# Attention scores from queries and keys split on VectorE, three single-pass products per pair of heads, keys in a ring

## The reference

```python
scores = q @ k.T / sqrt(64)                     # batch 2, 8 heads, 768 positions, head_dim 64
keep = (key < 4) | ((query - key >= 0) & (query - key < 128))
a = softmax(where(keep, scores, -1e9)); x = a @ v     # -> 1536 tokens x 512
x = moe_top2(x)     # 8 experts, 512 -> 1024 -> 512, noisy top-2 routing
x = moe_top1(x)     # 8 experts, 512 -> 1024 -> 512, top-1 routing
```

## Time and profile before

| what | value |
|---|---|
| median of 3 runs | 675.39 us |
| the profiled execution | 674.08 us, its span 672.0 us |
| TensorE busy | 639.0 us, 95% |
| VectorE busy | 329.8 us, 49% |
| ScalarE busy | 275.7 us, 41% |
| granted clock of TensorE over the span | 0.99 |
| attention stage | about the first 132 us |

### The profile page before, as it was taken

The page is one execution under the profiler, slowest core; times in us unless marked ns, Lnnn a source line. Parts: engine busy times, 40 slices in busy tenths (PEclk is TensorE's granted clock), DMA queues, the critical chain, the costliest instruction groups (busy, mean ns, idle before and its releaser), DMA issues.

```text
span 672.0 us, 11238 instructions
## 1 busy us (share of the span) xinstructions
PE 639.0 (95%) x3866; PEld 580.1 (86%) x3867; DVE 329.8 (49%) x681; ACT 275.7 (41%) x529; POOL 184.7 (27%) x199
## 2 busy tenths in 40 slices
PE   7989999899999999999999999999988999999981
PEld 6989999898999999999999999988767888788871
DVE  4466645588365526254361634467876222542220
ACT  5667866442344335252443523144516123522110
POOL 2500100117362533516144251201652121121010
PEclk9999999999999999999999999999998999999996
DMA  7867822263684646646355520724649211001000
GB/s 209 281 235 240 291 74 80 66 249 74 237 214 138 132 148 157 190 142 156 111 122 177 148 28 3 171 63 159 171 138 387 102 48 47 20 32 48 16 32 11
DMA packets 51089, 89.84 MB, mean 134 GB/s; under 512 B 7919, under 2 KB 14063, under 8 KB 51040
## 3 DMA queue, kind: packets, MB, share of 16 engines
q1 hardware_dynamic: 41872, 69.21, 31.0%
q0 software_dynamic: 9168, 19.97, 13.3%
HBM read 73.13 MB, written 17.02 MB: 134 GB/s over the span
## 4 chain that ended last, share of the span: by engine, by line
PE 82%; DVE 6%; DMA 3%; ACT 3%; issue 2%; SPq 1%; ACTq 0%; POOL 0%; DVEq 0%; POOLq 0%
PE banks L1060 6%; PE banks L1059 6%; PE banks L999 6%; PE banks L1078 6%; PE banks L1001 6%; PE banks L998 6%; PE banks L803 5%; PE banks L831 4%; PE banks L1377 3%; PE banks L1342 3%; PE banks L1347 3%; PE banks L1343 3%; PE banks L1373 3%; PE banks L1374 3%; PE banks L815 2%
## 5 line engine op out<-in xcount | busy, mean ns | idle before, releaser
L1833 DVE TENSOR_TENSOR split<-stage,split 128x2048 fp32r<-128x2048 f32 x32 | 73.3, 2290 | 41.9 <-ACT split L1463 41.8
L998 PE MATMUL banks<-xTs,split 128*128 128x416 f32 (+1 forms) x256 | 88.6, 350 | 0.0
L999 PE MATMUL banks<-xTs,split 128*128 128x416 f32 (+1 forms) x256 | 86.5, 342 | 0.0
L650 POOL DMA_INDIRECT x_moe<-rows,dst_idx x25 | 49.3, 1971 | 113.2 <-DVE rows L2285 112.2
L1059 PE MATMUL banks<-hTs,split 128*128 128x416 f32 x224 | 79.9, 357 | 0.0
L1060 PE MATMUL banks<-hTs,split 128*128 128x416 f32 x224 | 78.6, 351 | 0.0
L1598 ACT ACTIVATE hTs<-banks 128x416 fp32r<-128x416 f32 x56 | 29.0, 518 | 81.6 <-PE banks L1001 81.6
L1463 ACT ACTIVATE split<-stage 128x2048 fp32r<-128x2048 f32 x32 | 60.9, 1908 | 1.0 <-DMA stage<-w1a 1.0
L1720 ACT ACTIVATE hTs<-banks 128x512 fp32r<-128x512 f32 x28 | 16.5, 596 | 105.8 <-PE banks L1357 105.8
L1001 PE MATMUL banks<-xTs,split 128*128 128x416 f32 (+1 forms) x256 | 56.2, 340 | 0.0
L803 PE MATMUL banks<-k_sb,q_sb 128*128 128x260 f32 (+2 forms) x192 | 49.6, 384 | 3.5 <-DMA k_sb<-k_w 2.1
(11 more groups left out here) (371 smaller groups left out, 1308.3 us busy)
## 6 DMA issues: line engine op xcount, KB each, us to landing
stage<-w1a SPq DMA_DIRECT2D x16, 1024.0 KB, 7.6
stage<-w2a SPq DMA_DIRECT2D x16, 1024.0 KB, 5.4
k_sb<-k_w SPq DMA_DIRECT2D x12, 520.0 KB, 5.0
raw<-w1b SPq DMA_DIRECT2D x4, 1024.0 KB, 7.9
raw<-w2b SPq DMA_DIRECT2D x4, 1024.0 KB, 9.7
q_sb<-q_t SPq DMA_DIRECT2D x24, 128.0 KB, 3.1
x_attention<-rows SPq DMA_DIRECT2D x12, 256.0 KB, 6.1
split<-x_moe SPq DMA_DIRECT2D x12, 256.0 KB, 3.6
```

Of the source, the lines that this page charges most:

```text
L650: pool.indirect_dma_start(out=x_dram[1], out_offset=rows_at(dst_idx[0], early_dst, e, k), in_=y_lines(e, k), in_offset=None, compute_op=AL ...
L998: pe.matmul(psum, piece(slot, 0, o + c * FH), xTs[:, 0, c, 0:cols], start=(c == 0), stop=False)
L999: pe.matmul(psum, piece(slot, 1, o + c * FH), xTs[:, 0, c, 0:cols], start=False, stop=False)
L1833: dve.tensor_tensor(split_chunk(e % 2, 1, c), staged_chunk(e % 2, c), split_chunk(e % 2, 0, c).bitcast(F32), ALU.subtract).then_inc(low_do ...
```

## The change

Only the attention stage and what is loaded or prepared beside it changes.

- Block 0 keeps its fp32 products, on buffers of its own (`q_first`, `k_first`, 128 keys).
- From block 1 on, the scores of a pair are six products: for each of (queries high, keys high), (queries high, keys low) and (queries low, keys high), one product per head with 64 contraction rows. The one head lies in rows 0 to 63 of the array, the other in rows 64 to 127; no zeros are multiplied. The three products of a head add up in PSUM.
- VectorE makes the parts: a cast to fp32r and a subtraction, over 128x512, for the keys and again for the queries of each unit, one such split per odd step, a block ahead.
- The keys lie in a ring of two places of 132 columns (`ODD`), 128 keys and 4 sinks. Block i overwrites the place of block i-2, so only the new 128 keys of a unit are loaded (256 KB, not 520). There is one more mask, since the order of the two places changes with the block.
- A chunk of the first expert's weights is prepared in each of the blocks 2 to 5, not two in each of 2 and 3. Its low part is made in two halves at the steps 2 and 6; the last chunk's at step 6 of block 5 in one piece.
- The loads go to staging buffers and are issued earlier; the zeros are written in the blocks 4 and 5.

```diff
+ODD = P + SINK
+RING = 2 * ODD
...
+        with ExitStack() as first_block:
+            q_first = first_block.enter_context(nc.sbuf_tensor("q_first", [P, BATCH, PAIRS, 2, P], F32))
+            k_first = first_block.enter_context(nc.sbuf_tensor("k_first", [P, BATCH, PAIRS, P], F32))
...
-            k_sb = sb_early("k_sb", [P, BATCH, PAIRS, WIN])
+            k_ring = sb_early("k_ring", [P, BATCH, PAIRS, RING], F32R)
...
-            masks = sb_early("masks", [P, 3, WIN])
+            masks = sb_early("masks", [P, 4, WIN])
+            k_low_ring = sb_early("k_low_ring", [P, BATCH, PAIRS, RING], F32R)
+            q_high = sb_early("q_high", [P, BATCH, PAIRS, P], F32R)
+            q_low = sb_early("q_low", [P, BATCH, PAIRS, P], F32R)
+            q_raw = sb_early("q_raw", [P, BATCH, PAIRS, P])
+            k_raw = sb_early("k_raw", [P, BATCH, PAIRS, P])
...
+        def slot_of(i):
+            return ODD * (i % 2)
+
+        def keys_split(i, b):
+
+            return b + 1 if i == 0 else 2 * BATCH + 4 * i + 2 * b - 3
+
+        def queries_split(i, b):
+            return keys_split(i, b) + 1
...
             def load_unit(i, b):
-                q_unit = qT[bass.ds(i * BATCH + b, 1)].rearrange("a p j n -> (a p) j n")
-                for h in range(2):
-                    own = slice(h * HD, (h + 1) * HD)
-                    sp.dma_start(q_sb[own, b, :, h, :], q_unit[own]).then_inc(qk_in[b], 16)
-                sp.dma_start(k_sb[:, b], kW[bass.ds(i * BATCH + b, 1)].rearrange("a p j n -> (a p) j n")).then_inc(qk_in[b], 16)
+                q_unit, k_unit = qT[i * BATCH + b], kW[i * BATCH + b]
+                if i == 0:
+                    for h in range(2):
+                        own = slice(h * HD, (h + 1) * HD)
+                        sp.dma_start(q_first[own, b, :, h, :], q_unit[own]).then_inc(qk_in[b], 16)
+                    sp.dma_start(k_first[:, b], k_unit[:, :, 0:P]).then_inc(qk_in[b], 16)
+                    return
+                if i == 1:
+                    sp.wait_ge(scores_ready, 4 * b + 1)
+                else:
+                    sp.wait_ge(parts_split, queries_split(i - 1, b))
+                sp.dma_start(k_raw[:, b], k_unit[:, :, P:2 * P]).then_inc(qk_in[b], 16)
+                sp.dma_start(q_raw[:, b], q_unit).then_inc(qk_in[b], 16)
...
-            for i in (1, 2):
+            sp.wait_ge(setup_ready, 11)
+
+            for i in range(1, BLOCKS):
                 for b in range(BATCH):
+                    if i + 1 < BLOCKS:
+                        load_unit(i + 1, b)
                     store_x(i - 1, b)
-                next_block(i + 1)
+                    if b == 0 and i <= CHUNKS:
+                        load_first(sp, 0, i - 1)
...
+                if i == BLOCKS - 2:
+                    zero_rows(0, 8)
+                if i == BLOCKS - 1:
+                    zero_rows(8, TILES + 1)
...
                 b, pair, g = j // PAIRS, j % PAIRS, i * 8 + j
-                if pair == 0:
-                    pe.wait_ge(qk_in[b], i * 48 + 48)
+                if kind == 0 and pair == 0:
+                    pe.wait_ge(qk_in[b], 48)
+                if kind > 0 and pair == 0:
+                    pe.wait_ge(parts_split, queries_split(i, b))
                 if kind > 0 or j >= 2:
                     pe.wait_ge(masked, g * 2 - 2)
-                n = span(kind)
-                for h in range(2):
-                    mm = pe.matmul(S[:, j % 2, h, 0:n], q_sb[:, b, pair, h, :], k_sb[:, b, pair, 0:n], start=True, stop=True)
+                if kind == 0:
+                    for h in range(2):
+                        mm = pe.matmul(S[:, j % 2, h, 0:P], q_first[:, b, pair, h, :], k_first[:, b, pair, :], start=True, stop=True)
+                else:
+                    for n, (queries, keys) in enumerate(((q_high, k_ring), (q_high, k_low_ring), (q_low, k_ring))):
+                        for h in range(2):
+                            own = slice(h * HD, (h + 1) * HD)
+                            if kind == 1:
+                                window = keys[own, b, pair, :].rearrange("p (a n) -> p a n", a=2)[:, :, 0:P]
+                                psum = S[:, j % 2, h, 0:2 * P].rearrange("p (a n) -> p a n", a=2)
+                            else:
+                                window, psum = keys[own, b, pair, 0:WIN], S[:, j % 2, h, 0:WIN]
+                            mm = pe.matmul(psum, queries[own, b, pair, :], window, start=(n == 0), stop=(n == 2))
                 mm.then_inc(scores_ready, 1)
...
+            block_steps(2, 2, 2, {0: 0})
+            block_steps(3, 2, 2, {0: 1})
+            block_steps(4, 2, 2, {0: 2})
+            block_steps(BLOCKS - 1, 2, None, {4: 3})
...
+            def early_weights_low(c, half):
+
+                dve.wait_ge(high_done[c], 1)
+                columns = slice(c * CHUNK + (half == 1) * (CHUNK // 2), (c + 1) * CHUNK - (half == 0) * (CHUNK // 2))
+                low = dve.tensor_tensor(split[:, 0, 1, columns], stage[0][:, columns], split[:, 0, 0, columns].bitcast(F32), ALU.subtract)
+                if half != 0:
+                    low.then_inc(low_done[c], 1)
...
+            def split_keys(i, b):
+
+                at = slice(slot_of(i), slot_of(i) + P)
+                raw_keys = k_raw[:, b] if i else k_first[:, b]
+                if i > 0:
+                    dve.wait_ge(qk_in[b], 16 + 32 * (i + 1))
+                link(dve.tensor_copy(k_ring[:, b, :, at], raw_keys))
+                dve.tensor_tensor(k_low_ring[:, b, :, at], raw_keys, k_ring[:, b, :, at].bitcast(F32), ALU.subtract).then_inc(parts_split, 1)
+
+            def split_queries(i, b):
+                link(dve.tensor_copy(q_high[:, b], q_raw[:, b]))
+                dve.tensor_tensor(q_low[:, b], q_raw[:, b], q_high[:, b].bitcast(F32), ALU.subtract).then_inc(parts_split, 1)
+
+            def sink_keys():
+
+                dve.wait_ge(parts_split, BATCH)
+                dve.tensor_copy(k_ring[:, :, :, P:ODD], k_ring[:, :, :, 0:SINK]).then_inc(parts_split, 1)
+                dve.tensor_copy(k_low_ring[:, :, :, P:ODD], k_low_ring[:, :, :, 0:SINK]).then_inc(parts_split, 1)
...
-                    if pair == 1 and b < len(chunks):
-                        first_layer_low(0, chunks[b])
+                    if i == 0:
+                        if j in (0, 2):
+                            split_keys(0, j // 2)
+                        elif j == 3:
+                            sink_keys()
+                        elif j > 3:
+                            (split_queries if j % 2 else split_keys)(1, (j - 4) // 2)
+                    elif j % 2 and not last:
+                        (split_queries if j // 2 % 2 else split_keys)(i + 1, b)
+                    if j in chunks:
+                        early_weights_low(*chunks[j])
...
+            block_steps(2, 2, 2, {2: (0, 0), 6: (0, 1)})
+            block_steps(3, 2, 2, {2: (1, 0), 6: (1, 1)})
+            block_steps(4, 2, 2, {2: (2, 0), 6: (2, 1)})
...
+            block_steps(BLOCKS - 1, 2, None, {6: (3, None)})
...
```

More of the change, by code:

```diff
@@ L126, in build @@
         xTs = sb("xTs", [P, 2, DC, SLOTS], F32R)
-        with ExitStack() as early:
-            q_sb = early.enter_context(nc.sbuf_tensor("q_sb", [P, BATCH, PAIRS, 2, P], F32))
         hTs = sb("hTs", [P, 2, FC, SLOTS], F32R)
@@ L539, in iota @@
                           allow_small_or_imprecise_dtypes=True).then_inc(const_done, 1)
[L541 to L554 removed]
+            pool.memset(masks[:], 0.0).then_inc(setup_ready, 1)
+            pool.memset(ident[:], 0.0).then_inc(setup_ready, 1)
+            pool.wait_ge(setup_ready, 1)
+            select(masks[:, 0, SINK:P], -SINK, 1, [[-1, P - SINK]], MASKED, setup_ready)
+            pool.wait_ge(setup_ready, 2)
+            select(ident[:], 0, 1, [[-1, P]], 1.0, setup_ready, ALU.not_equal)
+            select(masks[:, 1, SINK:P], SINK - 1, -1, [[1, P - SINK]], MASKED, setup_ready)
+            select(masks[:, 1, P:2 * P], 0, 1, [[-1, P]], MASKED, setup_ready)
+            for odd in range(2):
+                select(masks[:, 2 + odd, ODD * (1 - odd):ODD * (1 - odd) + P], -1, -1, [[1, P]], MASKED, setup_ready)
+                select(masks[:, 2 + odd, ODD * odd:ODD * odd + P], 0, 1, [[-1, P]], MASKED, setup_ready)
+            pool.memset(rows[:, 5, :], 0.0).then_inc(setup_ready, 1)
             pool.memset(before[:], 1.0).then_inc(const_done, 1)
@@ L1510, in early_high_part, with block_steps @@
                                ACT.Copy).then_inc(x1_high, 1)
-            def block_steps(i, kind, next_kind, chunks=()):
+            def block_steps(i, kind, next_kind, chunks={}):
                 for j in range(8):
@@ L1525, in block_steps @@
                         x_copy(*((i, 0) if b else (i - 1, 1)))
-                    if pair == 0 and b < len(chunks):
-                        first_layer_high(0, chunks[b])
+                    if j in chunks:
+                        first_layer_high(0, chunks[j])
```

54 lines of the change are left out of this document (12 added, 42 removed).

## The result

The changed kernel took 701.5 us (median of 4 runs, 697.45 to 704.28) against 676.48 for the kernel before on the same chip (674.67 to 680.53): a ratio of 1.036, 95% interval 1.028 to 1.043. Forecast were 669.0 us and a range up to 680. The profiled execution took 704.28 us, its span is 702.5 (before: 674.08 and 672.0), and the mean granted clock of the span 0.94 where it was 0.99.

A forecast was written before the change was run, and what follows sets the result against it. TensorE was taken to bound the stage, busy all 10.60 us of a block 3 unit. Terms -9.5 + 2.5 + 1.5 - 0.6 - 0.7 = -6.8 us from 674.08 gave 667.3, median about 668.6, stated as 669.0; range 662 to 680.

The forecast's parts named there:

- the clock has nothing to give: Attention stage, block 3 unit: granted clock is 1.00 of the full 2.4 GHz, so no change in clock was priced.
- the slowest rival: Score sets: halves take turns and each shape change waits for the last product's whole record; T 1.05, 683.5 us, chance 0.09.
- T = 0.56 us: A set of scores on TensorE: 0.36 for pairs side by side plus 0.20 for shape changes, instead of 0.915 us.
- rivals 2 and 3: Score halves take turns: 678.1 or 680.7 us, chance 0.16; with shape changes waiting for a whole record: 683.5, chance 0.09.
- rival 1: Score sets: pairs run side by side and the shape change costs nothing; T 0.36, 664.2 us, chance 0.15.
- 9.18: TensorE's need in us per unit, after saving 1.42 on four sets of scores.
- VectorE loop of 9.84 us: Blocks 2 to 4: VectorE's work behind the logits and the way back to them, 9.28 + T, longer than TensorE's need.
- 0.76: Saving in us per unit in blocks 2 to 4, 10.60 - 9.84, as VectorE's loop limits it.
- 2.1: Block 5's saving in us: 1.42 a unit, with 0.7 taken off for the early choice of expert on VectorE.
- the last chunk's split: VectorE, step 6 of block 5: 2.4 us of work, costing nothing, or +1 if it delays the last normalizing.
- +2.5 less 0.6: Start: +2.5 us for splits and sink-key copies in block 0, -0.6 for first scores waiting for fewer key bytes.
- The wait of 1.5 us for block 2's keys: Block 1, step 1: VectorE's split waits for loads queued on SyncE; +1.5 us, between 0 and +3.

The follow-up runs named there:

- a_wait: Changed kernel with TensorE's wait for the sink values' parts moved from the start of block 2 to their first use; median 681.3 us, ratio 1.009.
- a_noselect: a_best with GpSimd's six masking instructions on the sink values cut to one column of 64 each; median 693.8 us, ratio 1.026.
- a_best: Changed kernel with the sink-value wait moved to first use and 5 unread products filling the first pause; median 702.6 us, no ratio.
- b_half: Kernel before, fp32 scores unsplit, each head's product reading only its own 64 rows; median 680.3 us, ratio 0.999.
- b_half_fill: Kernel before with unsplit fp32 scores on own 64 rows from block 1 on, plus 7 unread products before block 2; median 671.7 us, ratio 0.997.
- b_half14: Kernel before with unsplit fp32 scores on own 64 rows in blocks 1 to 4, plus 7 unread products before block 2; median 677.1 us, ratio 0.995.
- b_half3: Kernel before with unsplit fp32 scores on each head's own 64 rows from block 3 on only; median 673.6 us, ratio 1.002.
- b_gap: Kernel before with two fills of unused memory on VectorE, lengthening TensorE's pause before block 2; median 674.7 us, ratio 1.004.
- a_full: Changed kernel with scores over all 128 rows, so heads have no scores of their own; 675.7 us, one run, no ratio.
- b_half_gap: b_half with two memsets of an unread buffer on VectorE, lengthening TensorE's pause before block 2; median 692.4 us, ratio 1.016.
- a_feed2: Changed kernel with 2 unread full-height products ahead of each of 6 score sets of block 2; median 690.8 us, no ratio.

## Why the prediction was wrong

**The step that failed** is in its first paragraph: "the granted clock is 1.00 of the full 2.4 GHz, so the clock has nothing to give". I read that as a constant of the stage. It was a property of the work in it: full-height products with no pause over 1.4 us behind the first keys. The change touched both. It halved the rows of every set, and it put a split ahead of the low part of the sink values, for which TensorE waits. In my sum no term could be longer than its full-clock size, and the slowest rival was 683.5. The Trainium skill's page TensorE: Matmul & The Clock Gate, section What's actually happening, has the chip set the clock by how busy TensorE has lately been. By the busy share of the profile the long stretch at 0.50 doesn't agree with that: it was 60.00 of 60.00 us.

**The queue of VectorE.** I counted the splits' time in block 1 but never asked, of L1901, who waits behind it. Line L1947 (before: L1885) stands there and TensorE waits for it: 1.38 us became 2.71. Priced as a wait that is 1.3 us; the fall behind it cost 26.6.

**A set of scores.** T = 0.56 us was right to the hundredth (0.55 to 0.56). The pairs run side by side: in a_wait the products of two pairs start 0.12 apart.

```profile
62.31 0.28 PE L838 MATMUL banks<-k_low_ring,q_high 64*128 64x260 f32 x2
62.43 0.28 PE L838 MATMUL banks<-k_ring,q_low 64*128 64x260 f32 x2
```

So rivals 2 and 3, in which the halves take turns, are out, and rival 1 too. But the sum was short of a term: the change back to full height is paid in the turns behind the set, 0.15 us, on top of T. Set and turns fell by 0.21, not by 0.355, and TensorE needs 9.87 us a unit where I had 9.18 (the four changes back, and 0.08 on the sinks' product, make it 9.86). My VectorE loop of 9.84 us was close to right: the units of the blocks 2 to 4 take 9.97, and in every other unit of a_wait the chain runs through ScalarE and VectorE, past the half chunk, the masks and the split of the queries that I had counted, to the sinks' low part:

```profile
98.74 0.30 DVE sinkT L1933
99.05 0.04 issue
99.09 0.50 PE banks L883
```

TensorE arrives there 0.1 us earlier, so the two are level, and a faster set would have gained next to nothing more. That the saving of such a unit came out near the forecast, 0.63 against 0.76, is thus no sign that TensorE's sum was right. The unit before block 5 takes 10.79 us in a_wait, with 0.93 of them waiting for VectorE.

**What the stage gains at full clock.** From the first to the sixth sinks' product (block 2's first unit to block 4's second), before took 53.00 us (55.64 to 108.64) and a_wait 50.65 (59.23 to 109.88): 2.35 saved, where 5 x 0.76 = 3.8 was forecast. Block 5 took 20.42 and 20.38: nothing saved, where I had 2.1. Its units go through the early choice of expert on VectorE, and the last chunk's split of 2.20 us, priced at nothing or +1, is in the chain just ahead of the last sinks' product (152.90 in the changed kernel). By the count of the first section the change would save some 3 us in the stage at full clock, an estimate: 26.6 for the long fall and 6.8 x (17.6 - 9.97) / 17.6 = 2.9 for the short one off the 26.4. No run shows it: a_wait's fastest execution, with one fall of 13.7 us at the start, is 674.0 against a median before of 671.9.

**The start.** Block 1's first scores came at 17.67 us, +0.9 to before where +2.5 less 0.6 was forecast. The wait of 1.5 us for block 2's keys didn't show in the changed kernel; in a_noselect, where VectorE comes there sooner, it is 1.64 us. What did show there wasn't in the sum: while GpSimd masks the sink values, the same subtraction takes twice its time. Groups of VectorE in the first 30 us of the changed kernel, the second on keys split before GpSimd starts on that:

```profile
L1897 DVE TENSOR_TENSOR k_low_ring<-k_raw,k_ring 128x512 fp32r<-128x512 f32 x3 | 2.9, 962 | 0.1
...
L1897 DVE TENSOR_TENSOR k_low_ring<-k_first,k_ring 128x512 fp32r<-128x512 f32 x2 | 1.4, 693 | 0.1
```

**What stays open.** After the stage 4.1 us more are lost in the one profiled execution, where I had let the rest move along unchanged. The trace shows where: TensorE waits 3.43 us at 186.4, ahead of the first expert's early rows, and is at half clock from 190.6 to 194.0; the kernel before has neither. The same wait is 0.63 us in a_wait and 9.07 in a_best; I made no experiment on it. Nor is all of the spread the clock: two executions of b_half took 678.0 and 688.6 us at mean granted clocks of 0.981 and 0.982. Which of the small waits starts a fall and which doesn't isn't settled: in its profile a_wait passed one of 1.51 us at 49 us at full clock and b_half_fill one of 1.08 at 115, b_half14 fell with none over 0.45 in the 30 us before and b_half3 with none over 0.27. A change of the changed kernel that never falls wasn't found.

## What to carry to other kernels

A granted clock of 1.00 is a result of the work shown, not a given. Ask of every change whether it opens a wait of TensorE or replaces full-height products by ones on part of the array (among such sets the clock fell once with no wait over 0.27 us in the 30 us before), and give the half clock a rival with its own price, here a stage at 17.6 instead of 9.97 us a unit. Two products side by side in the array are worth their time less the change of shape, and that is paid at both ends, the way back in the instruction behind. When work is put into an in-order queue, look at what stands behind it and who waits for that. Filling a pause shows whether it was the cause, but look in the trace for the next fall before taking the time for the answer.

## What I had not expected of the hardware

- Sets of 64-row products hold the clock down. After a pause of 2.6 to 3.3 us the clock was at 0.50 for 3.4 us with 128-row sets (b_gap, a_full), some 31 with 64-row fp32 sets (b_half_gap), 61 with 64-row single-pass sets (changed kernel), though TensorE shows as busy all the time. With six full-height products of 128x512 among the 64-row sets it was back after 13.7 us (a_feed2).
- The same program falls in one execution and not in another: a_wait 674.0 and 705.7 us, b_half14 672.8 and 702.1.
- fp32 products of four passes run side by side in two halves too: 0.64 us for a pair, where the two full-height ones took 0.915.
- VectorE's cast of 128x512 went from 0.42 to up to 1.1 us and its subtraction from 0.69 to 1.50 while GpSimd's selects over 32x1024 ran; with selects of 32x16, done before most of the splits, they were 0.42 and 0.69. The Trainium skill's GPSIMD Engine Reference, section Specifications, lists contention with VectorE instructions of two SBUF inputs, as the subtraction is; it gives no size.
